# An fp32 attention and two-layer network kernel: first layer in blocks of 416 and 448 tokens, and GpSimd held at every third weight piece

## The chip, the cores and the metric

The kernel runs on one core of a Trainium2 chip. The metric is the device time of one execution in microseconds; lower is better. A core has TensorE (PE, matrix products), VectorE (DVE), ScalarE (ACT), GpSimd (POOL) and SyncE (SP, which here issues the DMAs). They run independently and wait for each other on semaphores.

## What is computed

```python
def reference(q, k, v, moe_w_gate, moe_w_val, moe_w_out, moe2_w_in, moe2_w_out, moe2_alpha):
    x = attention(q, k, v)                      # 4 x 8 heads, 576 positions, 64 wide
    x = x.transpose(0, 2, 1, 3).reshape(2304, 512)
    g = x @ moe_w_gate                          # 512 x 1536
    x = (g / (1 + exp(-g)) * (x @ moe_w_val)) @ moe_w_out
    h = x @ moe2_w_in                           # 512 x 2048
    return (max(h, 0) + moe2_alpha * min(h, 0)) @ moe2_w_out
```

The attention is the sum of two parts: one over keys and queries averaged in fours, and a local one over the neighbours less than 4 positions away. All of it is float32.

## The kernel before

**Precision.** Each factor of the large products is split into a high part in TensorE's reduced float32 form and a low part that holds the rest. A product takes three matmuls: high by high, high by low, low by high (PARTS and products(), L1092; outputs(), L1120; outputs2(), L1137). In all of them 128 x 128 of one operand are loaded first and the other streams past, as many columns as its width.

**Layer one** takes the 2,304 tokens in six blocks with widths SPANS (L70) and first tokens STARTS. A block has 12 steps, one for each 128 hidden units, and a step has three places: the gate product (12 matmuls), the value product (12 matmuls) and the output product of the step before (12 matmuls, accumulated in four banks of PSUM over the block). Between them the other engines work: ScalarE takes the tanh of the gate (L702), VectorE forms gated (L924) and hidden (L929), ScalarE copies hidden to h_hi (high_part, L674) and VectorE subtracts for h_lo (low_part, L914). The output product waits for h_lo_ready. The three weight pieces of step c are 3c (gate), 3c+1 (value) and 3c+2 (output), 36 in all, each 128 x 512.

**Weights.** SyncE loads a piece; for pieces 2 and up ScalarE copies its high part (first_weights_hi, L625), and GpSimd subtracts for the low part w_lo (low_part and split_rest, L520), in the order of the pieces. TensorE waits on w_ready, which counts them. GpSimd also normalises the attention weights of each unit (normalise, L536 and L539); how many pieces come ahead of each unit is set by `ready` in the loop over WORK.

**Attention** for 288 tokens (TB, half a sequence) and two heads is one unit. Four units make a half of x, rows k = 0 to 3 of the tiles x_hi and x_lo. The first half's units run at the start; those of the other seven are woven between the places of blocks 0 to 4, at the places of SCORED_IN, and that order is the same on every engine.

**The ring.** x_hi and x_lo hold, for each k, RING = 1,008 columns. Half a of x is written at the column that x_at() gives, block j reads from HOMES[j]. A block of 432 columns spans one and a half halves. Half 3 is the one of which block 2 reads the first 144 columns and block 3 the rest, and the two blocks lie in different parts of the ring: so it is written in two parts of 144 columns, 288 columns apart (x_at with a == 3).

**Layer two** reads x again from DRAM in six blocks of 384 tokens, in turns from the x2 tiles "even" and "odd". The odd pair shares its memory with x_hi and x_lo, the even pair with the attention's tiles behind y_sb. A block has 16 steps of 12 product matmuls of 384 columns and 9 output matmuls of 512 columns (L1137, where the weights stream and h is loaded).

The order is written by hand in each engine's block:

```python
SPANS = (288, 288, 432, 432, 432, 432)
HOMES = (432, 720, 0, 576, 0, 432)
...
            def split_rest(j):
                low_part(j, w_hi_copied, j - POOL_PIECES + 1)
...
                ready = min(max(EARLY_PIECES + unit.scored + 3, done), P1)
                for j in range(done, ready):
                    split_rest(j)
                done = ready
                normalise(unit.q, unit.q % PAIRS, 1)
```

Of the kernel before, what the change touches and what calls it, by code (L numbers as in the profile page):

```python
# [5 lines left out]
ALU = mybir.AluOpType  # L6
ACT = mybir.ActivationFunctionType
AX_X = mybir.AxisListType.X
F32 = mybir.dt.float32
# [12 lines left out]
TB = SEQ // 2  # L22
# [41 lines left out]

POOL_PIECES = 2
EARLY_PIECES = 6
EARLY_HI = 12
POOL_AVERAGES = 2
BANK = 512
SPANS = (288, 288, 432, 432, 432, 432)  # L70
STARTS = (0, 288, 576, 1008, 1440, 1872)
HOMES = (432, 720, 0, 576, 0, 432)
RING, WIDEST = 1008, max(SPANS)
NL1 = len(SPANS)
STEPS1 = NL1 * C1
TB2 = 384
# [9 lines left out]
class Unit:  # L86

    def __init__(self, q, block, place, following):
        narrow = SPANS[block] == TB
        self.q, self.scored = q, PLACES * block + place  # L90
# [28 lines left out]
def halves_for(j):  # L119

    return -(-(STARTS[j] + SPANS[j]) // TB)


def build(nc, qk, vwin, vsrc, w1, w2, alpha, out, y_t):
    with ExitStack() as ctx:
        def sem(name):
            return ctx.enter_context(nc.semaphore(name))

        def sb(name, shape, dt=F32, where=ctx):
            return where.enter_context(nc.sbuf_tensor(name, shape, dt))  # L130
# [4 lines left out]
        def bank(n):  # L135
            return ps[:, n * BANK:(n + 1) * BANK]

        y_ps = [[bank(m)[:, 0:span] for m in range(KC)] for span in SPANS]
        gate_ps, val_ps = [bank(4)[:, 0:span] for span in SPANS], [bank(5)[:, 0:span] for span in SPANS]

# [36 lines left out]
        with ExitStack() as early:  # L177
            sb("first_pieces", [128, EARLY_HI, PIECE], where=early)
            qk_early = [sb(f"qk_early{k}", [128, QK_W], where=early) for k in range(2, PAIRS)]
# [20 lines left out]
        with ExitStack() as first_x:  # L200
            x_hi = sb("x_hi", [128, KC, RING], F32R, where=first_x)
            x_lo = sb("x_lo", [128, KC, RING], F32R, where=first_x)
        with ExitStack() as second_x:
            x2_hi_odd = sb("x2_hi_odd", [128, KC, TB2], F32R, where=second_x)
            x2_lo_odd = sb("x2_lo_odd", [128, KC, TB2], F32R, where=second_x)
        sb("x_space", [128, 2 * KC * RING])
# [47 lines left out]
        x_f32 = ([x_f32_one] + x_f32_early, [x_f32_one] * PAIRS)  # L254
# [62 lines left out]
        x_hi_ready = sem("x_hi_ready")  # L317
        x_lo_ready = sem("x_lo_ready")
# [7 lines left out]
        h_lo_ready = sem("h_lo_ready")  # L326
# [12 lines left out]

        def x_at(ring, k, a):  # L340

            if a == 3:
                return ring[:, k, TB:3 * TB].rearrange("p (n s) -> p n s", n=2)[:, :, 0:TB // 2]
            first = (432, 720, 0, None, 720, 0, 288, 576)[a]
            return ring[:, k, first:first + TB]

        def x_from(tile, a):

            return tile[:, :].rearrange("p (n s) -> p n s", n=2) if a == 3 else tile[:, :]

        def second_layer(token_block):
            for j in range(NB2):
# [7 lines left out]
        def _(sp):  # L360
# [3 lines left out]
            def load_vwin(q, r):  # L364
                sp.dma_start(vwin_sb[0][r][:, :, :], vwin[bass.ds(q, 1), :, :, :].rearrange("a p t d -> (a p) t d")).then_inc(vwin_in[r], 16)
# [44 lines left out]
            def store_y(j):  # L410
                sp.wait_ge(y02_copied, 2 * j + 6)
                sp.wait_ge(y13_copied, 2 * j + 6)
                sp.dma_start(y_t[:, :, STARTS[j]:STARTS[j] + SPANS[j]].rearrange("k p s -> p k s"), y1_sb[j]).then_inc(y_stored, 16)

# [15 lines left out]
            for k in range(PAIRS):  # L430
# [3 lines left out]
                load_vwin(k, k)  # L434
            load_pieces(FIRST_LOADS, EARLY_PIECES)
            sp.dma_start(alpha_sb[:, :], alpha[:, :]).then_inc(alpha_in, 16)
# [3 lines left out]
            refill_vwin(0)  # L440
            load_pieces(EARLY_PIECES, EARLY_PIECES + 3)
            refill_vwin(1)
            load_pieces(EARLY_PIECES + 3, EARLY_LOADS)

# [37 lines left out]
        def _(pool):  # L482
# [34 lines left out]
            def low_part(at, hi_done, n):  # L517

                pool.wait_ge(hi_done, n)
                nc.gpsimd.tensor_tensor(w_lo[:, at, :], w_raw(at), w_hi[:, at, :].bitcast(F32), ALU.subtract).then_inc(w_ready, 1)  # L520

            def split_rest(j):
                low_part(j, w_hi_copied, j - POOL_PIECES + 1)

            def split_piece(j):
# [36 lines left out]
            for k in range(PAIRS - 1):  # L562
                split_x_lo(k)
            for j in range(POOL_PIECES, EARLY_PIECES):
                split_rest(j)
            done = EARLY_PIECES
            for unit in WORK:
                ready = min(max(EARLY_PIECES + unit.scored + 3, done), P1)
                for j in range(done, ready):
# [9 lines left out]
        def _(act):  # L579
# [35 lines left out]

            def split_x_hi(a, k, mode):
                act.wait_ge(x_added, PAIRS * a + k + 1)
                nc.scalar.copy(x_at(x_hi, k, a), x_from(x_f32[mode][k], a)).then_inc(x_hi_ready, 1)

# [119 lines left out]
        def _(dve):  # L741
# [91 lines left out]

            def split_x_lo(a, k, mode):
                dve.wait_ge(x_hi_ready, PAIRS * a + k + 1)
                nc.vector.tensor_tensor(x_at(x_lo, k, a), x_from(x_f32[mode][k], a), x_at(x_hi, k, a).bitcast(F32), ALU.subtract).then_inc(x_lo_ready, 1)

            def copy_out(j, steps):

# [126 lines left out]
        def _(pe):  # L966
# [176 lines left out]
            def first_block(j):  # L1143
                x_here = [ring[:, :, HOMES[j]:HOMES[j] + SPANS[j]] for ring in (x_hi, x_lo)]
                for p in range(PLACES):
# [82 lines left out]
```

## Time and profile before

| What | Before |
|---|---|
| median of 3 runs | 958.58 us (957.58 to 960.65) |
| the profiled execution's own time | 959.2 us |
| its span, from the first to the last instruction | 957.4 us |
| TensorE busy | 937.7 us, 98% of the span |
| VectorE / ScalarE / GpSimd busy | 504.4 / 279.6 / 140.9 us |
| mean granted clock of TensorE | 0.989 of full speed |

The profile is one execution, taken by the hardware. A row of a timeline says when an instruction (or several like it, x2) started, how long it took, and in brackets how long its engine had stood idle and what ended that. A matmul's recorded duration reaches into the next one's, so the spacing of their starts says what one costs. The chain of waits follows the work that ended last back to the start. L520 is line 520 of the kernel before.

### The profile page before, as it was taken

To read this page: it belongs to the slowest core of one execution; us is meant where nothing else is said; L and a number is where in the kernel's file an instruction comes from. 1 tells how busy PE (TensorE), PEld (TensorE's weight loads), DVE (VectorE), ACT (ScalarE), POOL (GpSimd) and SP (SyncE) were. 2 spreads that over 40 slices of the span, in tenths; PEclk is the share of its full clock that TensorE was granted. 3 is DMA by queue.
4 is the path that set the end of the run, shared out by engine and by line. 5 is a ranking of instruction groups with operands and counts; after the bars stand their busy time and mean duration, and the time that the engine had idled before them with its cause. 6 is when DMAs were issued, how large, how long until landed. Compare 5 with 4: busy or idle time off the path is not lost.

```text
span 957.4 us, 19243 instructions
## 1 busy us (share of the span) xinstructions
PE 937.7 (98%) x7944; PEld 861.9 (90%) x7944; DVE 504.4 (53%) x996; ACT 279.6 (29%) x707; POOL 140.9 (15%) x167
## 2 busy tenths in 40 slices
PE   4899999999999999999999999999999999999998
PEld 3899999999999999999999999998999998999897
DVE  8899777545466765444324245444444444444443
ACT  4566444322233433332134321111111111111111
POOL 7876010000011000000036430000000000000000
PEclk7899999999999999999999999999999999999999
DMA  9763323211122213110232320010100100100000
GB/s 270 240 199 105 104 81 108 78 48 41 41 70 84 90 66 92 54 34 2 75 128 100 120 72 1 12 55 1 66 0 1 66 2 0 66 1 1 34 1 34
DMA packets 31077, 63.24 MB, mean 66 GB/s; under 512 B 3344, under 2 KB 13584, under 8 KB 30992
## 3 DMA queue, kind: packets, MB, share of 16 engines
q1 hardware_dynamic: 30992, 62.02, 20.2%
q8 instruction: 64, 1.05, 0.4%
q14 instruction: 21, 0.17, 0.1%
HBM read 52.57 MB, written 9.44 MB: 65 GB/s over the span
## 4 chain that ended last, share of the span: by engine, by line
PE 95%; DVE 1%; DMA 1%; ACT 1%; SPq 1%; issue 0%; POOL 0%; DVEq 0%; ACTq 0%
PE ps L1092 53%; PE ps L1137 21%; PE ps L1120 16%; PE ps L1040 2%; PE ps L976 1%; DMA vsrc_early<-vsrc 1%; PE ps L986 1%; PE ps L1053 1%; PE ps L1024 1%; DVE h_lo L914 1%; SPq L369 0%; PE ps L1101 0%; ACT turned_early L604 0%; SPq L362 0%; ACT turned_one L604 0%
## 5 line engine op out<-in xcount | busy, mean ns | idle before, releaser
L674 ACT CAST h_hi<-hidden 128x384 fp32r<-128x384 f32 (+2 forms) x168 | 86.2, 513 | 426.0 <-DVE hidden L947 335.7
L1092 PE MATMUL ps<-x_hi,w_hi 128*128 128x432 f32 (+1 forms) x573 | 199.0, 347 | 0.0
L1092 PE MATMUL ps<-x_hi,w_lo 128*128 128x432 f32 (+1 forms) x573 | 193.2, 337 | 0.0
L1092 PE MATMUL ps<-x_lo,w_hi 128*128 128x432 f32 (+1 forms) x573 | 193.0, 337 | 0.0
L914 DVE TENSOR_TENSOR h_lo<-hidden,h_hi 128x384 fp32r<-128x384 f32 (+2 forms) x168 | 108.7, 647 | 72.3 <-ACT h_hi L674 72.3
L945 DVE TENSOR_SCALAR gated<-ps,alpha_sb 128x384 f32<-128x384 f32 x96 | 59.3, 618 | 165.3 <-PE ps L1092 165.3
L1137 PE MATMUL ps<-w_hi,h_hi 128*128 128x512 f32 x288 | 113.8, 395 | 0.4 <-DVE h_lo L914 0.4
L1137 PE MATMUL ps<-w_lo,h_hi 128*128 128x512 f32 x288 | 113.7, 395 | 0.0
L1137 PE MATMUL ps<-w_hi,h_lo 128*128 128x512 f32 x288 | 113.5, 394 | 0.0
L1092 PEld LDWEIGHTS ps<-x_hi,w_hi 128*128 128x128 f32 x573 | 107.9, 188 | 5.2 <-issue 0.2
L1092 PEld LDWEIGHTS ps<-x_lo,w_hi 128*128 128x128 f32 x573 | 107.9, 188 | 2.9
L1092 PEld LDWEIGHTS ps<-x_hi,w_lo 128*128 128x128 f32 x573 | 107.7, 188 | 3.0
L924 DVE SCALAR_TENSOR_TENSOR gated<-gated,ps 128x432 f32<-128x432 f32 (+1 forms) x72 | 39.5, 548 | 129.2 <-ACT gated L702 129.2
L520 POOL TENSOR_TENSOR w_lo<-w_home,w_hi 128x512 fp32r<-128x512 f32 x68 | 89.5, 1335 | 98.1 <-ACT w_hi L669 86.3
L1120 PE MATMUL ps<-h_hi,w_hi 128*128 128x432 f32 (+1 forms) x288 | 99.6, 346 | 2.6 <-DVE h_lo L914 2.5
L1120 PE MATMUL ps<-h_lo,w_hi 128*128 128x432 f32 (+1 forms) x288 | 97.4, 338 | 0.0
L1120 PE MATMUL ps<-h_hi,w_lo 128*128 128x432 f32 (+1 forms) x288 | 97.2, 338 | 0.0
L702 ACT ACTIVATE gated<-ps 128x432 f32<-128x432 f32 (+1 forms) x72 | 35.4, 491 | 145.8 <-PE ps L1092 145.8
L1137 PEld LDWEIGHTS ps<-w_lo,h_hi 128*128 128x128 f32 x288 | 54.1, 188 | 13.0
L929 DVE SCALAR_TENSOR_TENSOR hidden<-gated,ps 128x432 f32<-128x432 f32 (+1 forms) x72 | 39.8, 553 | 48.5 <-PE ps L1092 47.9
L1092 PE MATMUL ps<-x_lo_even,w_hi 128*128 128x384 f32 x192 | 64.9, 338 | 0.0
L1092 PE MATMUL ps<-x_hi_even,w_lo 128*128 128x384 f32 x192 | 64.8, 338 | 0.0
(140 smaller groups left out, 1431.8 us busy)
## 6 DMA issues: line engine op xcount, KB each, us to landing
w_home<-w SPq DMA_DIRECT2D x68, 256.0 KB, 3.8
qk<-qk SPq DMA_DIRECT2D x30, 436.0 KB, 3.7
vsrc_one<-vsrc SPq DMA_DIRECT2D x58, 144.0 KB
vwin<-vwin SPq DMA_DIRECT2D x30, 192.0 KB, 2.4
x_raw<-y_t SPq DMA_DIRECT2D x6, 768.0 KB, 5.5
out<-y_sb SPq DMA_DIRECT2D x5, 768.0 KB, 4.0
y_t<-y_sb SPq DMA_DIRECT2D x4, 864.0 KB, 4.6
y_t<-y_sb SPq DMA_DIRECT2D x2, 576.0 KB, 4.0
```

What stands on the lines that cost most here:

```text
L520: nc.gpsimd.tensor_tensor(w_lo[:, at, :], w_raw(at), w_hi[:, at, :].bitcast(F32), ALU.subtract).then_inc(w_ready, 1)
L674: nc.scalar.copy(h_hi[r][:, 0:width], hidden[r][:, 0:width]).then_inc(h_hi_ready, 1)
L702: nc.scalar.activation(gated[:, 0:span], gate_ps[j], ACT.Tanh, scale=0.5).then_inc(tanh_ready, 1)
L914: nc.vector.tensor_tensor(h_lo[r][:, 0:width], hidden[r][:, 0:width], h_hi[r][:, 0:width].bitcast(F32), ALU.subtract).then_inc(h_lo_ready, 1)
L924: nc.vector.scalar_tensor_tensor(out=gated[:, 0:span], in0=gated[:, 0:span], scalar=1.0, in1=gate_ps[j], op0=ALU.add, op1=ALU.mult).then_i ...
L929: nc.vector.scalar_tensor_tensor(out=hidden[r][:, 0:span], in0=gated[:, 0:span], scalar=0.5, in1=val_ps[j], op0=ALU.mult, op1=ALU.mult).th ...
L945: nc.vector.tensor_scalar(gated[:, 0:TB2], pre_ps[r], 0.0, alpha_sb[:, c:c + 1], ALU.min, ALU.mult).then_inc(gated_ready, 1)
L976: last = nc.tensor.matmul(local_ps(mode, k, e)[GK * i:GK * i + SCORED, t * GK:(t + 1) * GK], qk_sb[mode][k][rows, first:first + SCORED], q ...
L1040: nc.tensor.matmul(att_ps(mode, k, r)[rows, t * ROW_Q:(t + 1) * ROW_Q].rearrange("p (i q) -> p i q", q=GQ), vwin_sb[mode][k][keys, t, rows ...
L1092: mm = nc.tensor.matmul(out_ps, w[:, piece, 128 * k:128 * k + 128], x_parts[low][:, k, :], start=(k == 0 and n == 0), stop=(k == KC - 1 an ...
L1120: mm = nc.tensor.matmul(y_ps[j][m], w[:, piece, 128 * m:128 * m + 128], (h_lo if low else h_hi)[c % 2][:, 0:SPANS[j]], start=(c == 0 and n ...
L1137: mm = nc.tensor.matmul(banks[m], (h_lo if low else h_hi)[c % 2][:, 128 * m:128 * m + 128], w[:, piece, :], start=(c == 0 and n == 0), sto ...
```

## The change

Blocks 2 to 5 of layer one have 416, 448, 448 and 416 tokens. The ring has 1,024 columns, the homes move, and half 3 now lies in one piece: block 2 reads columns 160 to 576, the first 288 of them half 2 and the last 128 the head of half 3, and block 3 goes on at 576. A spacer of 16 numbers (64 bytes) moves the odd x2 tiles. The buffers that have the width of the widest block (h_hi, h_lo, gated, hidden, y_sb) become 448 wide, and with them the tiles behind move. On GpSimd, each piece from 9 on whose number is divisible by 3 also waits for h_lo of step (piece - 9) / 3.

```diff
+PACED = 9
-SPANS = (288, 288, 432, 432, 432, 432)
-STARTS = (0, 288, 576, 1008, 1440, 1872)
-HOMES = (432, 720, 0, 576, 0, 432)
-RING, WIDEST = 1008, max(SPANS)
+SPANS = (288, 288, 416, 448, 448, 416)
+STARTS = (0, 288, 576, 992, 1440, 1888)
+HOMES = (448, 736, 160, 576, 0, 448)
+HALVES_AT = (448, 736, 160, 448, 736, 0, 288, 576)
+RING, WIDEST = 1024, max(SPANS)
...
         with ExitStack() as second_x:
+            sb("odd_start", [128, 16], where=second_x)
             x2_hi_odd = sb("x2_hi_odd", [128, KC, TB2], F32R, where=second_x)
...
         def x_at(ring, k, a):
 
-            if a == 3:
-                return ring[:, k, TB:3 * TB].rearrange("p (n s) -> p n s", n=2)[:, :, 0:TB // 2]
-            first = (432, 720, 0, None, 720, 0, 288, 576)[a]
-            return ring[:, k, first:first + TB]
-
-        def x_from(tile, a):
-
-            return tile[:, :].rearrange("p (n s) -> p n s", n=2) if a == 3 else tile[:, :]
+            return ring[:, k, HALVES_AT[a]:HALVES_AT[a] + TB]
...
             def split_rest(j):
+                if j >= PACED and j % 3 == 0:
+                    pool.wait_ge(h_lo_ready, (j - PACED) // 3 + 1)
                 low_part(j, w_hi_copied, j - POOL_PIECES + 1)
...
-                nc.scalar.copy(x_at(x_hi, k, a), x_from(x_f32[mode][k], a)).then_inc(x_hi_ready, 1)
+                nc.scalar.copy(x_at(x_hi, k, a), x_f32[mode][k][:, :]).then_inc(x_hi_ready, 1)
```

GpSimd's order from piece 2 on, in block 0 of layer one, before (w_lo is the low part of one piece; local_one and down belong to the normalising of a unit):

```order
L520 TENSOR_TENSOR w_lo<-w_home,w_hi 128x512 [waits w_hi_copied] x8
L536 TENSOR_TENSOR local_one<-local_one,row_inv 128x192 [waits inv_ready]
L539 TENSOR_TENSOR down<-down,row_inv 72x8x36
L520 TENSOR_TENSOR w_lo<-w_home,w_hi 128x512 [waits w_hi_copied] x6
L536 TENSOR_TENSOR local_one<-local_one,row_inv 128x192 [waits inv_ready]
L539 TENSOR_TENSOR down<-down,row_inv 72x8x36
L520 TENSOR_TENSOR w_lo<-w_home,w_hi 128x512 [waits w_hi_copied] x6
```

And with the change:

```order
L516 TENSOR_TENSOR w_lo<-w_home,w_hi 128x512 [waits w_hi_copied] x7
L516 TENSOR_TENSOR w_lo<-w_home,w_hi 128x512 [waits w_hi_copied,h_lo_ready]
L534 TENSOR_TENSOR local_one<-local_one,row_inv 128x192 [waits inv_ready]
L537 TENSOR_TENSOR down<-down,row_inv 72x8x36
L516 TENSOR_TENSOR w_lo<-w_home,w_hi 128x512 [waits w_hi_copied] x2
L516 TENSOR_TENSOR w_lo<-w_home,w_hi 128x512 [waits w_hi_copied,h_lo_ready]
L516 TENSOR_TENSOR w_lo<-w_home,w_hi 128x512 [waits w_hi_copied] x2
L516 TENSOR_TENSOR w_lo<-w_home,w_hi 128x512 [waits w_hi_copied,h_lo_ready]
L534 TENSOR_TENSOR local_one<-local_one,row_inv 128x192 [waits inv_ready]
L537 TENSOR_TENSOR down<-down,row_inv 72x8x36
L516 TENSOR_TENSOR w_lo<-w_home,w_hi 128x512 [waits w_hi_copied] x2
L516 TENSOR_TENSOR w_lo<-w_home,w_hi 128x512 [waits w_hi_copied,h_lo_ready]
L516 TENSOR_TENSOR w_lo<-w_home,w_hi 128x512 [waits w_hi_copied] x2
```

The order of the work is the same; the eighth piece of the first run (piece 9), the third and the sixth of the second (pieces 12 and 15) and so on now wait for h_lo_ready too.

TensorE's order where block 1's last outputs end and block 2's first gate product begins, before:

```order
L1120 MATMUL ps<-h_hi,w_hi 128x288
L1120 MATMUL ps<-h_lo,w_hi 128x288
L1120 MATMUL ps<-h_hi,w_lo 128x288
L1092 MATMUL ps<-x_hi,w_hi 128x432 [waits gated_ready,w_ready,x_lo_ready,x_hi_ready]
L1092 MATMUL ps<-x_lo,w_hi 128x432
```

And with the change:

```order
L1118 MATMUL ps<-h_hi,w_hi 128x288
L1118 MATMUL ps<-h_lo,w_hi 128x288
L1118 MATMUL ps<-h_hi,w_lo 128x288
L1090 MATMUL ps<-x_hi,w_hi 128x416 [waits gated_ready,w_ready,x_lo_ready,x_hi_ready]
L1090 MATMUL ps<-x_lo,w_hi 128x416
```

Nothing moved there; the matmuls of block 2 have 416 columns, not 432, and wait for the same semaphores. The line numbers are those of the changed kernel.

## Rows read from the trace of the kernel before

**Rows 1.** The page: the span, and each engine's busy time.

```profile
span 957.4 us, 19243 instructions
...
PE 937.7 (98%) x7944; PEld 861.9 (90%) x7944; DVE 504.4 (53%) x996; ACT 279.6 (29%) x707; POOL 140.9 (15%) x167
```

**Rows 2.** Waits of TensorE, 20 to 958 us: total, times, longest us.

```profile
PE ps L1120 <- DVE h_lo L914: 2.5, 2, 1.8
```

**Rows 3.** Timeline of TensorE, 26 to 58 us: start, duration, [idle before <- releaser].

```profile
37.74 0.37 PE L1120 MATMUL ps<-h_hi,w_hi 128*128 128x288 f32 x1 [0.75 <-DVE h_lo L914]
...
43.54 0.30 PE L1092 MATMUL ps<-x_hi,w_lo 128*128 128x288 f32 x1
45.63 0.37 PE L1120 MATMUL ps<-h_hi,w_hi 128*128 128x288 f32 x1 [1.80 <-DVE h_lo L914]
45.84 0.29 PE L1120 MATMUL ps<-h_lo,w_hi 128*128 128x288 f32 x1
```

**Rows 4.** Timeline of VectorE, 24 to 62 us: h_lo of steps 0 to 3.

```profile
36.28 1.31 DVE L914 TENSOR_TENSOR h_lo<-hidden,h_hi 128x288 fp32r<-128x288 f32 x1 [0.41 <-ACT h_hi L674]
...
41.19 4.30 DVE L914 TENSOR_TENSOR h_lo<-hidden,h_hi 128x288 fp32r<-128x288 f32 x1
...
49.21 1.31 DVE L914 TENSOR_TENSOR h_lo<-hidden,h_hi 128x288 fp32r<-128x288 f32 x1 [0.41 <-ACT h_hi L674]
...
53.73 2.22 DVE L914 TENSOR_TENSOR h_lo<-hidden,h_hi 128x288 fp32r<-128x288 f32 x1
```

**Rows 5.** Timeline of GpSimd, 0 to 110 us.

```profile
36.00 2.74 POOL L520 TENSOR_TENSOR w_lo<-w_home,w_hi 128x512 fp32r<-128x512 f32 x2 [0.22 <-ACT w_hi L625]
39.08 0.51 POOL L536 TENSOR_TENSOR local_one<-local_one,row_inv 128x192 f32<-128x192 f32 x1 [0.35 <-DVE row_inv L811]
...
40.17 5.00 POOL L520 TENSOR_TENSOR w_lo<-w_home,w_hi 128x512 fp32r<-128x512 f32 x4
48.92 2.74 POOL L520 TENSOR_TENSOR w_lo<-w_home,w_hi 128x512 fp32r<-128x512 f32 x2 [3.75 <-ACT w_hi L625]
52.01 0.51 POOL L536 TENSOR_TENSOR local_one<-local_one,row_inv 128x192 f32<-128x192 f32 x1 [0.34 <-DVE row_inv L811]
...
56.04 2.68 POOL L520 TENSOR_TENSOR w_lo<-w_home,w_hi 128x512 fp32r<-128x512 f32 x2 [0.41 <-ACT w_hi L625]
```

**Rows 6.** Timeline of GpSimd, 41.5 to 43.9 us: pieces 11 and 12.

```profile
41.42 2.53 POOL L520 TENSOR_TENSOR w_lo<-w_home,w_hi 128x512 fp32r<-128x512 f32 x2
```

**Rows 7.** Timeline of ScalarE, 25 to 60 us: the high part of piece 12.

```profile
41.70 0.62 ACT L625 CAST w_hi<-w_home 128x512 fp32r<-128x512 f32 x1
```

**Rows 8.** Chain of waits, 0 to 115 us: start, us, what, matmuls.

```profile
47.46 1.59 PE ps L1092 x12
...
51.69 1.82 PE ps L1120 x12
```

**Rows 9.** Chain of waits, 470 to 500 us, block 5 of layer one.

```profile
470.16 4.69 PE ps L1092 x24
...
498.38 1.76 PE ps L1092 x9
```

**Rows 10.** Chain of waits, 565 to 690 us, layer two.

```profile
568.99 2.12 PE ps L1092 x12
571.11 2.08 PE ps L1137 x9
...
610.99 2.12 PE ps L1092 x12
...
619.38 2.11 PE ps L1092 x12
...
678.27 2.11 PE ps L1092 x12
```

**Rows 11.** Groups of instructions by form: count | busy us, mean ns | idle.

```profile
L1092 PE MATMUL ps<-x_hi,w_hi 128*128 128x432 f32 x384 | 140.4, 366 | 0.0
...
L1120 PE MATMUL ps<-h_hi,w_hi 128*128 128x432 f32 x192 | 69.8, 364 | 0.0
```

More of the change, by code:

```diff
@@ L835, in split_x_lo @@
                 dve.wait_ge(x_hi_ready, PAIRS * a + k + 1)
-                nc.vector.tensor_tensor(x_at(x_lo, k, a), x_from(x_f32[mode][k], a), x_at(x_hi, k, a).bitcast(F32), ALU.subtract).then_inc(x_lo_ready, 1)
+                nc.vector.tensor_tensor(x_at(x_lo, k, a), x_f32[mode][k][:, :], x_at(x_hi, k, a).bitcast(F32), ALU.subtract).then_inc(x_lo_ready, 1)
             def copy_out(j, steps):
```

## The prediction

> **What bounds the kernel now.** I read the page first. TensorE is busy for 937.7 of 957.4 us [rows 1], and its multiplications make up nearly the whole chain of waits. So a change pays in one of two ways only: TensorE stops waiting somewhere, or a matmul follows the one before it sooner. I then read what TensorE waits for after the first 20 us. Of the waits that the change touches only one is large: before its output matmuls it waits for the low part of the hidden activation (h_lo), 2.5 us in two waits of which the longest is 1.8 [rows 2]. TensorE's own timeline gives the place: a product matmul starts at 43.54, the next one, an output matmul of step 1, at 45.63; the smaller wait of 0.75 us ends at 37.74, in step 0 [rows 3]. VectorE's timeline shows why: h_lo of step 1 starts at 41.19 and takes 4.30 us, where those of steps 0, 2 and 3 take 1.31, 1.31 and 2.22 [rows 4]. GpSimd's timeline fits to the hundredth: it forms the low parts of four weight pieces back to back from 40.17 to 45.17, and h_lo ends 0.31 us later, at 45.49. Around the shorter ones it runs only pairs of pieces, from 36.00 and from 48.92 [rows 5]. Both engines subtract two tiles that lie in SBUF.
>
> The Trainium skill describes this: in "SBUF — State Buffer", section "Who interferes with whom", a VectorE instruction with two SBUF inputs and a GpSimd instruction that reads SBUF exclude each other, and whoever issues first holds the shared ports for its whole instruction. The trace agrees that one waits, but not on how long: by that rule h_lo would wait for the piece in progress only.
>
> **The hold on GpSimd.** Pieces 9, 12, 15 and so on wait for h_lo of steps 0, 1, 2. The changed order shows the first burst cut into seven pieces and a held one, the second into two, a held one, two, a held one.
>
> *Piece 12, step 1.* Pieces 10 and 11 run as before; piece 12 is the third of the four. Piece 11 starts at 41.42 and two pieces from there take 2.53 us [rows 6], so it ends at about 41.42 + 1.27 = 42.69. There GpSimd now stands still, h_lo needs its 0.31 us, and is ready at about 43.0 in place of 45.49. TensorE could start its output matmul one spacing of 0.13 us after 43.54, at 43.67: h_lo is then ready 0.6 us early and the wait is gone. The gain is 45.63 - 43.67 = 1.96 us, and the first matmul after the wait is followed after 0.21 us, not 0.13, which gives 0.08 more [rows 3]: **2.0 us**. It isn't given back in the next step: VectorE gains 2.5 us there, more than TensorE's 2.0, so its lead grows.
>
> *What stands behind the waiting piece.* Piece 12 itself was waiting for ScalarE's high part until 41.70 + 0.62 = 42.32 [rows 7]; held, it runs from about 43.1 to 44.4, piece 13 to 45.7. Piece 12 is a gate weight of step 4, and TensorE starts that step's gate only behind the outputs that it begins at 51.69 [rows 8], 49.7 after the gain: over 5 us are left. Behind piece 13 come piece 14, which waited for ScalarE until 48.92 anyway [rows 5], and the normalising of the next attention unit.
>
> *The other holds.* Piece 9 is held until h_lo of step 0 ends at 37.59 instead of starting near 37.2: either way it ends before the normalising at 39.08 [rows 5]; cost 0, gain 0. The 0.75 us of step 0 stays, because pieces 6 to 8 aren't held and h_lo waits for piece 8. Piece 15 is the second of the pair at 48.92, held until 50.52 [rows 4, 5]; it then ends near 51.9, and GpSimd's next work starts at 52.01 [rows 5]. Piece 18 started at 56.04, after h_lo of step 3 had ended at 55.95: already late enough, and pieces 16 and 17 hold that h_lo up as before. This pair of steps repeats to piece 35, so the later holds change nothing. If TensorE's slack there were gone, each h_lo of 2.22 us would cost up to 1.8 us; in the trace TensorE doesn't wait for one.
>
> **Widths 416 and 448.** The instruction counts stay; 4 x (288 + 144) = 1,728 matmuls of 432 columns, three times 384 and three times 192 [rows 11], become 864 of 416 and 864 of 448, with the same sum of columns. What I need is the spacing of two new widths, and no row has it. The rows give for 432 columns four steps of 36 matmuls in 498.38 - 470.16 = 28.22 us, 196.0 ns each, 0.454 ns a column [rows 9]; for 384 columns 2.12 / 12 = 176 ns, 0.459 a column, for 512 columns 2.08 / 9 = 231 ns, 0.451 [rows 10]; for 288 columns 1.59 / 12 = 132.5 ns, 0.460 [rows 8]. A pair now takes 392.0 ns. At the cheapest rate it would take 864 x 0.4514 = 390.0 (864 x -2.0 ns = -1.7 us), at the dearest 864 x 0.460 = 397.4 (+4.7 us). I take 0: both new widths lie 16 columns from 432, the nearest row, and a slope cancels in the pair. Block by block it doesn't cancel: block 2 gets shorter by 432 x 7 ns = 3 us and block 3 longer by as much, with attention units of unchanged size in both. VectorE and ScalarE are 16 columns shorter or longer with it, which their idle time hides.
>
> **New places.** Adding up the tiles, x_hi began at a multiple of 128 bytes; its rows for the four k were 4,032 bytes apart, so every second one started on an odd multiple of 64 bytes, and with the homes 432 and 720 the other ones. Now rows are 4,096 apart and all homes are multiples of 128 bytes. In layer two the x2 tiles, both at even multiples of 64 before, now both start on odd ones; the spacer of 16 numbers does that for the odd tile and costs no time. The nearest rows are the two x2 tiles of before, whose starts differ by 128 bytes modulo 256: even block, ten steps in 610.99 - 568.99 = 42.00 us, 4.200 each; odd block, fourteen in 678.27 - 619.38 = 58.89, 4.206 each [rows 10]. A place moves the time by a thousandth, either way: I take 0. The lower bound is that the narrow matmuls come down to the rate of the cheapest row: 1,152 of 384 columns by 176 - 173.3 = 2.7 ns (3.1 us) and 864 of 288 columns by 2.5 ns (2.2 us); the upper bound stands under the rivals.
>
> The copies of half 3 of x lose their split form and keep 288 columns; DMAs stay in number and order. All of that costs 0, hidden by idle time of VectorE and ScalarE.
>
> **Sum.** 959.2 us (the profiled execution) - 2.0 + 0 + 0 = 957.2. The median of the runs, 958.58, is 0.6 lower than that execution, so I predict **956.6**. A measurement of this kernel tells about 0.3%, 2.9 us, from no change; this forecast is below that.
>
> **The rivals.**
> *Matmuls follow each other sooner as well.* With even places every matmul of layer one and the narrow ones of layer two could approach the cheapest rate: at most 1.7 + 3.1 + 2.2 = 7.0 us, with the hold 9.0, 949.6; at half of it 953.1. For it: 0.459 against 0.451 a column is no law of width alone. Against it: the two x2 places differ by 0.006 us a step. Chance 0.35, for 950 to 955.5.
> *The hold frees nothing.* If h_lo waits for one instruction only, its 4.30 us has another cause and piece 12's hold gains 0: 958.6. This is the skill's lock taken at its word. The end 0.31 us behind a burst of four speaks against it; chance 0.07.
> *Slower: a product pays for its odd start.* If each matmul that reads x2 from an odd multiple of 64 bytes took up 64 bytes more, 16 columns at 0.459, that is 7.3 ns x 1,152 = 8.5 us: 956.6 + 8.5 = 965.1. It decides once the 96 steps of layer two grow by over 2.0 / 96 = 0.02 us each. Against it: block 5 read odd and even rows by turns, at 0.454 a column. The same skill page, under "Specifications (TRN2)", names lines of 16 bytes, by which no place here would matter; no run here shows it. Chance 0.07.
> *Slightly dearer widths*, up to +2.9 us: 957.5 to 959.5, chance 0.08.
>
> **How the numbers follow.** The forecast, 955.5 to 957.5, has 0.43. The range of 8 in 10 goes from 952.0 to 959.5: it leaves out the slower rival and the far end of the faster one. Faster by over 0.3% means under 955.7: 0.35 and a little of the forecast, 0.38. Slower: 0.07. Same: 0.55.
>
> **What would show it.** Right: h_lo of step 1 takes about 1.8 us and TensorE no longer waits before the outputs of step 1; a wait of about 0.75 remains in step 0; 12 outputs of 416 columns take about 2.27 us and of 448 about 2.44; steps of layer two stay at 4.20. Wrong: h_lo of step 1 still takes 4 us; TensorE waits for a low part of a weight; or the steps of layer two move by 0.02 us or more, which makes the places, not the hold, the larger part.

## The result, and the profile after

| What | Before | After |
|---|---|---|
| median | 958.64 us (957.58 to 960.65, 4 runs) | 951.05 us (950.30 to 951.81, 4 runs) |
| the profiled execution's own time | 959.2 us | 951.09 us |
| its span | 957.4 us | 949.0 us |
| TensorE busy | 937.7 us | 931.3 us |

The ratio is 0.9918, with an interval of 0.9900 to 0.9936: 7.6 us faster, where 2.0 were forecast. The page of the changed kernel, its span and the busy times, beside [rows 1]:

```profile
span 949.0 us, 19252 instructions
...
PE 931.3 (98%) x7944; PEld 857.6 (90%) x7944; DVE 504.5 (53%) x996; ACT 279.3 (29%) x707; POOL 140.2 (15%) x167
```

TensorE issues the same 7,944 matmuls and is busy for 6.4 us less. Waits that go away don't change busy time much; matmuls that follow each other sooner do.

First the place that the forecast was about. TensorE's waits for h_lo after 20 us, in all, times, longest (us), beside [rows 2] (L1118 and L1135 are outputs() and outputs2() now):

```profile
PE ps L1118 <- DVE h_lo L912: 0.9, 1, 0.9
...
PE ps L1135 <- DVE h_lo L912: 0.5, 1, 0.5
```

VectorE's timeline, steps 0 to 3 and the first instruction of the next attention units, beside [rows 4]:

```profile
35.69 1.31 DVE L912 TENSOR_TENSOR h_lo<-hidden,h_hi 128x288 fp32r<-128x288 f32 x1 [0.42 <-ACT h_hi L672]
...
40.81 1.82 DVE L912 TENSOR_TENSOR h_lo<-hidden,h_hi 128x288 fp32r<-128x288 f32 x1
...
47.01 1.33 DVE L912 TENSOR_TENSOR h_lo<-hidden,h_hi 128x288 fp32r<-128x288 f32 x1 [0.41 <-ACT h_hi L672]
48.63 1.09 DVE L805 TENSOR_SCALAR row_padded<-row_sum 128x8 f32<-128x8 f32 x1
...
51.76 2.22 DVE L912 TENSOR_TENSOR h_lo<-hidden,h_hi 128x288 fp32r<-128x288 f32 x1
...
60.81 1.09 DVE L805 TENSOR_SCALAR row_padded<-row_sum 128x8 f32<-128x8 f32 x1
```

The hold did what was said: h_lo of step 1 takes 1.82 us instead of 4.30, and the wait of 1.80 us [rows 3] is gone. Only the one of step 0 is left, 0.94 us.

Then layer two. The chain of waits of the changed kernel there (start, us, what; L1090 is products(), L1135 outputs2()), beside [rows 10]:

```profile
566.86 2.08 PE ps L1090 x12
568.94 2.05 PE ps L1135 x9
...
624.73 2.08 PE ps L1090 x12
626.81 2.05 PE ps L1135 x9
```

The first pair lies in an even block, the second in an odd one, and they are alike. From 566.86 to 624.73 there are 14 steps, 57.87 us, 4.134 each, where before they took 4.200 and 4.206. Over 96 steps this is about 96 x 0.07 = 6.7 us.

I took the start of every block from TensorE's matmuls in both traces, and the differences of these starts add up to the whole:

| Stretch | Before | After | Difference |
|---|---|---|---|
| up to the first full product of block 0 | 31.90 | 31.02 | -0.9 |
| block 0 (steps 0 to 11) | 68.86 | 68.41 | -0.45 |
| block 1 | 72.58 | 72.59 | 0 |
| blocks 2 to 5, together | 374.23 | 373.81 | -0.4 |
| layer two, from its first matmul to the end of the kernel | 409.85 | 403.21 | -6.6 |

Together they are -8.4 us, the difference of the two spans, 957.4 and 949.0. In layer two the first five blocks, 67.2 to 67.5 us each before and 66.1 to 66.3 after, and the last one with its tail get shorter by 1.06 to 1.15 each.

The first full product also starts 0.6 to 0.9 us sooner or later between executions of kernels that are the same up to there; I claim nothing of that row. Block 0 repeats better when it is counted from the first matmul of products() in it, the last quarter of its first gate product (29.74 and 29.15 us). It then takes 71.01 us before and 70.28 with the change, 0.7 less. In the five kernels of this document that have no hold it takes 70.98 to 71.04, in the six with the hold on every third piece 70.23 to 70.36.

TensorE's granted clock was lower at the start of the profiled execution before (0.74 in its first 24 us, 0.83 in the next 24, against 1.0 with the change). It has no part in the rows below the first: the kernel with the hold alone, next section, was granted 1.0 throughout, and a block of its layer two takes 67.21 to 67.46 us, as before.

So two questions stood: what in layer two got cheaper, though nothing in it was changed but addresses; and why block 0, which lost a wait of 1.8 us, is only 0.5 to 0.7 shorter.

### The profile page after: what moved, and what is told of

The parts are those of the page before. It is cut to its first block, busy times and chain, and to the rows that moved or that the text cites. A ratio compares the mean times of both kernels' runs of the same rounds, so it can differ in the third digit from the quotient of the medians.

```text
span 949.0 us, 19252 instructions
## 1 busy us (share of the span) xinstructions
PE 931.3 (98%) x7944; PEld 857.6 (90%) x7944; DVE 504.5 (53%) x996; ACT 279.3 (29%) x707; POOL 140.2 (15%) x167
## 4 chain that ended last, share of the span: by engine, by line
PE 90%; DVE 4%; issue 2%; ACT 1%; DMA 1%; SPq 1%; POOL 0%; DVEq 0%; ACTq 0%
PE ps L1090 50%; PE ps L1135 21%; PE ps L1118 14%; PE ps L1038 1%; PE ps L974 1%; DMA vsrc_early<-vsrc 1%; PE ps L984 1%; PE ps L1051 1%; PE ps L1022 1%; DVE v_d_one L768 1%; DVE row_padded L805 1%; DVE gated L922 0%; DVE h_lo L912 0%; DVE neg_max L796 0%; SPq L365 0%
## 5 line engine op out<-in xcount | busy, mean ns | idle before, releaser
L672 ACT CAST h_hi<-hidden 128x384 fp32r<-128x384 f32 (+3 forms) x168 | 86.3, 513 | 419.6 <-DVE hidden L945 329.4
L1090 PE MATMUL ps<-x_hi,w_hi 128*128 128x416 f32 (+2 forms) x573 | 199.1, 347 | 0.0
L1090 PE MATMUL ps<-x_lo,w_hi 128*128 128x416 f32 (+2 forms) x573 | 193.1, 337 | 0.0
L1090 PE MATMUL ps<-x_hi,w_lo 128*128 128x416 f32 (+2 forms) x573 | 193.1, 337 | 0.0
L912 DVE TENSOR_TENSOR h_lo<-hidden,h_hi 128x384 fp32r<-128x384 f32 (+3 forms) x168 | 106.4, 633 | 72.2 <-ACT h_hi L672 72.2
L1135 PE MATMUL ps<-w_hi,h_hi 128*128 128x512 f32 x288 | 112.3, 390 | 0.5 <-DVE h_lo L912 0.5
L1135 PE MATMUL ps<-w_hi,h_lo 128*128 128x512 f32 x288 | 112.6, 391 | 0.0
L1090 PEld LDWEIGHTS ps<-x_hi,w_hi 128*128 128x128 f32 x573 | 107.6, 188 | 5.5 <-DVE gated L922 0.3
L1135 PE MATMUL ps<-w_lo,h_hi 128*128 128x512 f32 x288 | 112.4, 390 | 0.0
L1090 PEld LDWEIGHTS ps<-x_hi,w_lo 128*128 128x128 f32 x573 | 107.7, 188 | 3.3
L1090 PEld LDWEIGHTS ps<-x_lo,w_hi 128*128 128x128 f32 x573 | 107.8, 188 | 2.8
L1118 PE MATMUL ps<-h_hi,w_hi 128*128 128x288 f32 (+2 forms) x288 | 99.7, 346 | 0.9 <-DVE h_lo L912 0.9
L1118 PE MATMUL ps<-h_lo,w_hi 128*128 128x288 f32 (+2 forms) x288 | 96.9, 336 | 0.0
L1118 PE MATMUL ps<-h_hi,w_lo 128*128 128x288 f32 (+2 forms) x288 | 96.9, 336 | 0.0
L927 DVE SCALAR_TENSOR_TENSOR hidden<-gated,ps 128x288 f32<-128x288 f32 (+2 forms) x72 | 39.8, 552 | 48.3 <-PE ps L1090 47.6
L1090 PE MATMUL ps<-x_hi_odd,w_lo 128*128 128x384 f32 x192 | 64.5, 336 | 0.0
L1090 PE MATMUL ps<-x_hi_even,w_lo 128*128 128x384 f32 x192 | 64.5, 336 | 0.0
```

Of the source, the lines that this page charges most:

```text
L672: nc.scalar.copy(h_hi[r][:, 0:width], hidden[r][:, 0:width]).then_inc(h_hi_ready, 1)
L912: nc.vector.tensor_tensor(h_lo[r][:, 0:width], hidden[r][:, 0:width], h_hi[r][:, 0:width].bitcast(F32), ALU.subtract).then_inc(h_lo_ready, 1)
L927: nc.vector.scalar_tensor_tensor(out=hidden[r][:, 0:span], in0=gated[:, 0:span], scalar=0.5, in1=val_ps[j], op0=ALU.mult, op1=ALU.mult).th ...
L1090: mm = nc.tensor.matmul(out_ps, w[:, piece, 128 * k:128 * k + 128], x_parts[low][:, k, :], start=(k == 0 and n == 0), stop=(k == KC - 1 an ...
L1118: mm = nc.tensor.matmul(y_ps[j][m], w[:, piece, 128 * m:128 * m + 128], (h_lo if low else h_hi)[c % 2][:, 0:SPANS[j]], start=(c == 0 and n ...
L1135: mm = nc.tensor.matmul(banks[m], (h_lo if low else h_hi)[c % 2][:, 128 * m:128 * m + 128], w[:, piece, :], start=(c == 0 and n == 0), sto ...
```

## The experiments

**What lies where.** The places below are the starts of tiles in bytes modulo 256, from adding up the tiles in the order of their allocation. They count the first tile, the weights' high part, as 128, which no trace shows; the distances between tiles don't depend on it. Before: h_hi of the two buffers at 128 and 64, h_lo at 0 and 192 (each is 1,728 bytes long, 64 short of a multiple of 256); x2 of even blocks at 0, of odd blocks at 128. After: all four h tiles at 128 (1,792 bytes each, a multiple of 256), x2 of both at 192. The split weights are at 128 in both. The change thus moved two things in layer two, the streamed x2 and the loaded h.

**The hold alone.** The kernel before with the hold added.

```diff
             def split_rest(j):
+                if j >= 9 and j % 3 == 0:
+                    pool.wait_ge(h_lo_ready, (j - 9) // 3 + 1)
```

> The kernel before with the hold on GpSimd alone; widths, ring and tiles as before. Theory 'VectorE takes over': in the changed kernel the steps of block 0 behind the freed wait grew from about 5.8 to 6.4 us every second step, and the chain there runs on VectorE. So the hold gives 2.0 us in step 2 and loses most of it again by the end of block 0: 0.3 to 0.9 us faster in all, about 958.0, block 0 about 0.5 us shorter. Rival 'the full wait': nothing is given back, 2.0 us faster, 956.6, the steps behind it keep their 5.8 to 6.0 us.

Measured: 958.58 us (957.59 to 959.70, 11 runs) against 959.91 for before (20 runs), ratio 0.9986, interval 0.9977 to 0.9996: 1.3 us, a little more than was expected. TensorE's wait goes, as in the changed kernel. Of it block 0 keeps 0.6 (68.27 us), as expected; in block 1 one step takes 0.6 more than before, and VectorE waits 2.2 us for a transfer of queries and keys there (1.7 before). The hold is not where the 7.6 us come from.

**The change without the hold.** The changed kernel, and only the wait on GpSimd taken out.

```diff
             def split_rest(j):
-                if j >= PACED and j % 3 == 0:
-                    pool.wait_ge(h_lo_ready, (j - PACED) // 3 + 1)
```

> The changed kernel without the hold; widths and places of the change stay. Theory 'places carry it': layer two keeps its steps of 4.13 us, and only the hold's net part is lost: 951.4 to 952.0, and step 1's h_lo takes about 4.3 us again. Rival 'the hold matters more': 953 or more.

Measured: 952.36 us (5 runs) against 959.91, ratio 0.9928 (0.9914 to 0.9942), -7.55 us. Steps of layer two are 4.13 us, block 0 is 69.16. Nearly the whole gain is there without the hold. The ratio, 0.9928 beside 0.9918 for the change, leaves about 1 us for it, within the noise of both; block 0, 0.75 longer than in the changed kernel, says the same more surely.

**Only x2 moved.** The kernel before, its widths and ring unchanged, with spacers so that both x2 pairs start at 192.

```diff
         with ExitStack() as second_x:
+            sb("odd_start", [128, 16], where=second_x)
...
+        sb("even_start", [128, 48])
         x2_hi = [sb("x2_hi_even", [128, KC, TB2], F32R), x2_hi_odd]
```

> The kernel before with the two x2 tiles of layer two moved, by spacers of 64 and 192 bytes, to the places modulo 256 bytes that they have in the changed kernel; nothing else moves. Theory 'the streaming operand's place': the 12 product matmuls fall from 2.11 to about 2.08 us, the 9 output matmuls, which stream weights that have not moved, stay at 2.08 to 2.10; steps near 4.17, 3 us faster. Rival 'the loaded operand's place' (h): no change, 4.20. Rival 'the pace of one group carries on into the next': both groups fall, steps 4.13, 6.7 us faster.

Measured: 956.53 us (9 runs) against 959.91, ratio 0.9967 (0.9956 to 0.9979), -3.4 us. Its chain in layer two:

```profile
600.48 2.10 PE ps L1139 x9
602.58 2.08 PE ps L1094 x12
604.66 2.08 PE ps L1139 x9
```

The 12 products are down from 2.11 to 2.08 us; the 9 outputs still take 2.10 and 2.08 by turns, as the h buffers take turns. A step is 4.17.

**Only h moved.** The kernel before, with each h tile 16 numbers longer, so that all four start at 128; x2 stays at 0 and 128.

```diff
-        h_hi = [sb(f"h_hi{r}", [128, WIDEST], F32R) for r in range(2)]
-        h_lo = [sb(f"h_lo{r}", [128, WIDEST], F32R) for r in range(2)]
+        h_hi = [sb(f"h_hi{r}", [128, WIDEST + 16], F32R) for r in range(2)]
+        h_lo = [sb(f"h_lo{r}", [128, WIDEST + 16], F32R) for r in range(2)]
...
+        sb("even_start", [128, 64])
         x2_hi = [sb("x2_hi_even", [128, KC, TB2], F32R), x2_hi_odd]
```

> The kernel before with 64 bytes more behind each of the four h tiles, so that all four start at the same place modulo 256 bytes as in the changed kernel; the x2 tiles keep their places modulo 512 bytes. Theory 'streaming operand': layer two's 9 output matmuls, which only load h, stay at 2.08 to 2.10, and the 12 products too; layer one's output matmuls, which stream h, get a little faster, under 1 us in all. Rival 'loaded operand': the 9 outputs fall to 2.05 and the products stay at 2.11: steps 4.16, 3.5 us faster.

Measured: 956.17 us (6 runs) against 959.91, ratio 0.9961 (0.9947 to 0.9975), -3.7 us. Its chain, first in an even block, then in an odd one:

```profile
601.64 2.10 PE ps L1093 x12
603.75 2.06 PE ps L1138 x9
...
618.31 2.10 PE ps L1093 x12
620.41 2.08 PE ps L1138 x9
```

Now the outputs are cheaper, 2.06 and 2.08, and no longer go by turns; the products stay at 2.10. Blocks 2 to 5 of layer one, where h streams, are 373.5 us together, 0.7 less than before. There are two effects, mainly one of x2 on the products and one of h on the outputs. By the traces, layer two is 3.1 us shorter with x2 moved, 2.8 with h moved, and 6.6 with both (the next experiment), 0.7 more than the sum.

**Both moved, nothing else.** The last two edits together: widths 432, ring of 1,008, no hold.

```diff
+            sb("odd_start", [128, 16], where=second_x)
...
+        h_hi = [sb(f"h_hi{r}", [128, WIDEST + 16], F32R) for r in range(2)]
+        h_lo = [sb(f"h_lo{r}", [128, WIDEST + 16], F32R) for r in range(2)]
...
+        sb("even_start", [128, 112])
```

> The kernel before with both moves of the two experiments before: x2 tiles and h tiles at the places modulo 256 bytes of the changed kernel, widths 432, no hold. Theory 'places carry layer two': products 2.08 and outputs 2.05 us, steps 4.13, layer two 6.7 us shorter than before; 953 against 959.9. Rival 'the two moves overlap': steps stay near 4.16, 956.

Measured: 951.94 us (5 runs) against 959.67 for before (9 runs), ratio 0.9924 (0.9911 to 0.9938), -7.7 us. Its chain in layer two is that of the changed kernel, 4.13 a step:

```profile
568.02 2.08 PE ps L1094 x12
570.10 2.05 PE ps L1139 x9
572.15 2.08 PE ps L1094 x12
```

Blocks 2 to 5 take 373.5 us with 432 columns, 373.3 with 416 and 448 and no hold. So the widths, the ring and the homes together bring nothing that can be measured (they were not tried one by one): a few numbers more in the allocation do.

**Other places for x2.** The changed kernel with x2 of even and odd blocks at 0 and 128, and at 64 and 0; h stays at 128. One execution each, read by their traces.

```diff
-            sb("odd_start", [128, 16], where=second_x)
+            sb("odd_start", [128, 32], where=second_x)
...
+        sb("even_start", [128, 32])
```

(the second; the first takes odd_start out and puts an even_start of 16)

> The changed kernel with the even x2 tiles at 0 and the odd ones at 128 bytes modulo 256 (both at 192 in the changed kernel; the weights that are loaded against them lie at 128). h is left where the change has it. Theory 'odd multiples of 64 are the good ones for x2': steps above 4.13 in both kinds of block, products near 2.11. Rival 'any one place for all is good': steps stay at 4.13 in both.

> The changed kernel with the even x2 tiles at 64 and the odd ones at 0 bytes modulo 256. Theory 'odd multiples of 64': even blocks keep products of 2.08 and steps of 4.13, odd blocks have dearer ones, 4.16 or more. Rival 'only 192 is good': both dearer.

Measured: 955.07 and 953.12 us. The chain of the second kernel, first an even block (x2 at 64), then an odd one (at 0):

```profile
608.10 2.12 PE ps L1091 x12
610.22 2.04 PE ps L1136 x9
612.26 2.10 PE ps L1091 x12
614.37 2.06 PE ps L1136 x9
```

A step takes 4.16 us with x2 at 64 or at 0, 4.19 at 128 (the odd blocks of the first, 66.99 / 16), 4.13 at 192. The same place at 0 or at 128 costs the same in either kernel's products, 2.10 to 2.11. Where x2 lies also shifts the outputs behind them by up to 0.04 us, so only the whole step compares. Both expectations had a theory that odd multiples of 64 are the cheap places, and the second experiment refutes it: at 64 a step costs as much as at 0, and of the four places only 192 is cheap.

The first kernel has the same places modulo 256 as the one in which only h moved, but not modulo 512 (counted from the weights, its even x2 tiles start 384 bytes past a multiple of 512, there 128), and widths, ring and hold differ. Its blocks of layer two take 66.99 and 66.56 us by turns, as there. That speaks for the places modulo 256 as the ones to look at.

**Other places for h.** The changed kernel with h at 192 (spacer of 16 numbers) and at 64 (spacer of 48); x2 stays at 192.

```diff
         sb("x_space", [128, 2 * KC * RING])
+        sb("h_start", [128, 16])
         h_hi = [sb(f"h_hi{r}", [128, WIDEST], F32R) for r in range(2)]
...
+        sb("even_start", [128, 112])
```

> The changed kernel with all four h tiles 64 bytes further, at 192 modulo 256; x2 stays at 192. Theory 'one place for all four h tiles is what counts': outputs of layer two stay at 2.05. Rival 'the loaded operand must lie at the same place as the streaming weights, 128': outputs rise to 2.08 or more.

> The changed kernel with the four h tiles at 64 modulo 256 bytes (128 in the change), x2 at 192, the weights at 128. In layer two the products stream x2 from 64 bytes past their loaded operand's place and are cheapest so; the outputs stream the weights. Theory 'streaming 64 bytes past the loaded operand is the cheap place in both': outputs at or below 2.05. Rival 'equal places are the cheap ones for the outputs': outputs 2.08 or more.

Measured: 954.47 us for 192, 957.89 for 64, one execution each. The chain of the one with h at 192:

```profile
584.92 2.10 PE ps L1137 x9
587.02 2.08 PE ps L1092 x12
```

At 192 and at 64 the outputs take 2.10 us, at 128 2.05, with the same products. The theory that what counts is by how much the streamed operand starts past the loaded one falls with these two. What is left for the outputs is that of the three places tried (all four tiles at 0 was not) h is cheapest at the very place of the weights that stream past it, 128. For the products that rule doesn't hold: their weights are loaded from 128 too, x2 is cheapest at 192, and at 128 it is dearest. Of the 6.8 us that the kernel with h at 64 is slower than the changed one, layer two is 3.8 and blocks 2 to 5 are 0.5. The other 2.4 are in its start, where TensorE waits 4.9 us for a normalised tile (2.9 in the changed kernel), and one execution doesn't tell whether a place has a part in that.

**The hold on piece 12 only.** The other question, block 0. In the changed kernel VectorE is slower there than TensorE: row_padded, which it does once for every two steps, is at 48.63 and 60.81, 12.18 apart, and takes 1.09 us, where it took 0.87 before. Its GpSimd timeline shows what is new beside it, beside [rows 5]:

```profile
48.42 1.28 POOL L516 TENSOR_TENSOR w_lo<-w_home,w_hi 128x512 fp32r<-128x512 f32 x1 [0.40 <-DVE h_lo L912]
```

That is piece 15, held until h_lo ends, and started just ahead of row_padded, which then ends 0.02 us after it. The experiment leaves the hold on piece 12 alone.

```diff
             def split_rest(j):
-                if j >= PACED and j % 3 == 0:
-                    pool.wait_ge(h_lo_ready, (j - PACED) // 3 + 1)
+                if j == 12:
+                    pool.wait_ge(h_lo_ready, 2)
```

> The changed kernel with the hold on piece 12 alone; pieces 9, 15, 18, 21 and so on go as soon as their high part is there. Theory 'the held second piece of a pair delays VectorE': in the changed kernel row_padded (two engines, one port) takes 1.10 us in place of 0.87 once per attention unit, because the held piece starts 0.2 us later; without it the period of VectorE's chain in block 0 falls from 12.17 to about 11.96 us, block 0 gets 0.8 us shorter, total 950.2 to 950.6 beside 951.3 for the change. Rival: the 12.17 us have another cause, block 0 stays at 68.4.

Measured: 950.04 us (4 runs) against 958.94 for before (7 runs), ratio 0.9908 (0.9892 to 0.9925). VectorE's timeline:

```profile
48.58 0.87 DVE L805 TENSOR_SCALAR row_padded<-row_sum 128x8 f32<-128x8 f32 x1
...
60.55 0.87 DVE L805 TENSOR_SCALAR row_padded<-row_sum 128x8 f32<-128x8 f32 x1
```

The two steps take VectorE 11.97 us, and block 0 is 67.14 us instead of 68.41, 69.19 instead of 70.28 by the other count. The medians of the two kernels lie within each other's noise; block 0, which repeats within 0.15 us by that count, tells them apart. Of the 1.1 us 0.9 lie in the last four pairs of steps, where the holds on pieces 15, 21 and so on act, and 0.2 in steps 0 and 1, where the one on piece 9 does. Without any hold block 0 takes 70.99. So the hold on piece 12 wins 1.8 us there, and the other holds cost 1.1 of them.

**Holds where VectorE needs them.** If GpSimd's bursts are what makes VectorE slow, holds at better pieces should bring block 0 down to what TensorE needs. Pieces 10, 16, 22 and on wait for the h_lo of the step at hand, pieces 12, 18, 24 and 30 for neg_max of the unit, and one piece less comes ahead of each unit.

```diff
-                if j >= PACED and j % 3 == 0:
-                    pool.wait_ge(h_lo_ready, (j - PACED) // 3 + 1)
+                if j >= 10 and j % 6 == 4:
+                    pool.wait_ge(h_lo_ready, (j - 10) // 3 + 2)
+                if j >= 12 and j % 6 == 0:
+                    pool.wait_ge(neg_max_ready, PAIRS + (j - 12) // 6 + 2)
...
-                ready = min(max(EARLY_PIECES + unit.scored + 3, done), P1)
+                ready = min(max(EARLY_PIECES + unit.scored + 2, done), P1)
```

> The changed kernel with other holds: pieces 10, 16, 22, 28, 34 wait for the h_lo that collides with them (steps 1, 3, 5, 7, 9), pieces 12, 18, 24, 30 for the row maxima of the next attention unit, and one piece more goes behind each normalising (9, 15, 21, ...). Theory 'VectorE's waits for the shared port set block 0': h_lo of the odd steps falls from 2.2 to about 0.5 us, the chain on VectorE gets shorter than TensorE's 11.8 us for two steps, block 0 falls to 66.6 to 67.4 us, total about 950. Rival 'it only moves the waits': other VectorE instructions wait for the pieces instead, block 0 stays at 68.4 or grows.

Measured: 949.15 us (948.50 to 950.49, 4 runs) against 958.94, ratio 0.9900 (0.9884 to 0.9917). VectorE's timeline, h_lo of steps 1 and 3 and the unit's row_padded:

```profile
39.66 0.59 DVE L914 TENSOR_TENSOR h_lo<-hidden,h_hi 128x288 fp32r<-128x288 f32 x1
...
49.80 0.58 DVE L914 TENSOR_TENSOR h_lo<-hidden,h_hi 128x288 fp32r<-128x288 f32 x1
...
57.91 0.88 DVE L807 TENSOR_SCALAR row_padded<-row_sum 128x8 f32<-128x8 f32 x1
...
69.68 0.88 DVE L807 TENSOR_SCALAR row_padded<-row_sum 128x8 f32<-128x8 f32 x1
```

Two steps now take 11.77 us, which is TensorE's own pace (5.77 + 5.99 for the two kinds of step), and block 0 is 66.65 us, 1.8 less than in the changed kernel. One piece also comes behind the normalising that came ahead of it, so this run doesn't tell what the holds bring without that. VectorE's busy time, with the same instructions, falls by 10 us, which are waits for GpSimd inside its own instructions:

```profile
PE 928.6 (98%) x7944; PEld 856.9 (91%) x7944; DVE 494.4 (52%) x996; ACT 280.1 (30%) x707; POOL 141.5 (15%) x167
```

It has the lowest median of all that ran, 9.8 us under before. Its interval overlaps with that of the changed kernel, 0.9900 to 0.9936, which was timed against other runs of before; block 0 tells them apart.

## Why the prediction was wrong, step by step

**What bounds it, and the hold: right in its mechanism, wrong in what it keeps.** The wait of 1.8 us went, by the numbers given: h_lo of step 1 takes 1.82 us, TensorE waits for no low part of a weight, and step 2 takes 5.88 us instead of 7.90, 2.0 less. Block 0 gives back 1.4 us of it (steps 4 to 11 take 48.56 us instead of 47.40, and steps 0 and 1 together 9.85 instead of 9.65). Two steps of the prediction failed there.

The larger one is "*The other holds*", priced at 0. In the kernel with the hold on piece 12 alone steps 4 to 11 take 47.69 us, and steps 0 and 1 9.64: so the other holds cost 0.9 and 0.2. Piece 15 was checked against "GpSimd's next work starts at 52.01". But that work waits for VectorE's row_inv [rows 5], and row_inv for row_padded, which piece 15 holds up: 0.22 us more in every period of VectorE, 12.18 instead of 11.96. The hold on piece 9 does the same to the first row_padded, 1.10 us instead of 0.87.

The smaller one is "It isn't given back in the next step: VectorE gains 2.5 us there, more than TensorE's 2.0, so its lead grows." The lead, from the end of h_lo to the start of its outputs, grew to 0.7 us in step 1, but in step 2 it was 0.85 us where before it was 1.10: neg_max, which met no piece before and took 0.17 us, took 0.82 beside the held piece 12 and piece 13. And row_padded of the kernel before comes every 11.96 us:

```profile
50.82 0.87 DVE L807 TENSOR_SCALAR row_padded<-row_sum 128x8 f32<-128x8 f32 x1
...
62.78 0.87 DVE L807 TENSOR_SCALAR row_padded<-row_sum 128x8 f32<-128x8 f32 x1
```

VectorE needed 11.96 us for two steps where TensorE needs 11.76. Behind its long wait TensorE had VectorE's lead to live on: 1.60, 1.44, 1.30 and 1.20 us in steps 3, 5, 7 and 9 before. With the change it is 1.08 and then 0.92 in each, and the slower engine sets the pace. The last four pairs of steps of block 0 take 11.81, 11.80, 11.85 and 11.94 us before, 12.02, 12.18, 12.17 and 12.19 after, and 11.83 to 11.97 in the kernel with the hold on piece 12 alone. That is 1.2 us given back, of which 0.3 go to this step and 0.9 to the other holds. I had checked each held piece against GpSimd's next work and against TensorE, but not against what VectorE does beside it.

**Widths 416 and 448: right.** 12 outputs of 416 columns take 2.24 us and of 448 2.44, 24 products 4.48 and 4.86, as in these rows of the changed kernel's chain (block 4, then block 5), beside 4.69 for 24 products of 432 [rows 9]:

```profile
441.98 4.86 PE ps L1090 x24
446.84 2.44 PE ps L1118 x12
...
472.07 4.48 PE ps L1090 x24
476.55 2.24 PE ps L1118 x12
```

24 products of either width are 9.34 us together, two times 4.69 is 9.38: 1.7 ns a pair less. Over the four blocks little of that is left: they are 0.4 us shorter in all, and the two kernels without a hold and with h at 128 that differ in the widths, the ring and the homes have 373.5 and 373.3 us there. Zero was the right value.

**New places: the step that made the number wrong.** "A place moves the time by a thousandth, either way: I take 0." It moved a step of layer two by 1.6%, 6.6 us in all against a term of 0. Three things were wrong in it. The two x2 places of before, 0 and 128, were taken as a sample of what places do; at those two the products happen to cost the same (2.105 and 2.106 us in one kernel with h at 128), while 192 gives 2.081 and 64 gives 2.120. Second, only the streamed x2 was costed. That h_hi and h_lo move too stood in the change ("with them the tiles behind move") and has no term in the sum, though they are loaded for 864 matmuls and it is worth 2.8 us alone and 3.5 on top of the move of x2. Third, the lower bound let only narrow matmuls get cheaper and held those of 512 columns for the cheapest row, so that the nearest row was taken for a floor; they fell from 2.08 to 2.10 us for nine down to 2.05, which is 3.8 of the 6.6 us. The products gave the other 2.8.

The rule of the Trainium skill in "SBUF — State Buffer", section "Specifications (TRN2)", that a line has 16 bytes, was cited for the view that no place here would matter. The runs disagree with that reading: every place tried is a multiple of 64 bytes, and a step goes from 4.13 to 4.21 us with it.

**The rivals.** "Matmuls follow each other sooner as well" (0.35) is the one whose range came true, in part by luck. Its reason, "even places", can't be that of layer two, where x2 moved to odd multiples of 64. Of its 3.9 us for layer one (1.7 + 2.2) the traces show 0.4 in blocks 2 to 5 and none in block 1; of its 3.1 for the products of layer two they show 2.8; and the 3.8 of the outputs it left out. As to the slower rival, "Slower: a product pays for its odd start" had the sign turned round, since x2 on an odd multiple of 64 is the cheapest in the one case (192) and no dearer in the other (64). "The hold frees nothing" fell with the run of the hold alone. It was what the Trainium skill says in "SBUF — State Buffer", section "Who interferes with whom", taken at its word: whoever issues first holds the shared ports for its whole instruction. The prediction read that as: and no longer. The measured waits go both ways. In step 1 h_lo waited through four pieces that followed each other without a gap (4.30 us), and with the burst cut after two it took 1.82; in step 3 it waited through both pieces of a pair. But in steps 0 and 2 it waited for one piece only, as the rule has it, though the next one stood ready: in step 2 of the kernel before h_lo ends at 50.52, 0.31 us behind the first piece of its pair (50.21), and the second takes 1.50 us instead of 1.28. The prediction read only the longer waits.

**The signs.** The prediction named the one that came: steps of layer two that move by 0.02 us or more make the places the larger part. They moved by 0.07. Of the right signs, 12 outputs of 416 columns take 2.24 us where 2.27 were said, and the wait in step 0 is 0.94 where 0.75 were said.

**The range.** It ended at 952.0, 0.95 above the result. The faster rival, by its own price, reached to 949.6, and the range cut that end off; after the two terms above that had no row behind them, it should have stayed in.

## What to carry to other kernels

A change of buffer widths moves every tile behind it: list, before predicting, each operand that TensorE loads or streams with its start modulo 256 bytes before and after, and treat an unseen place as unknown, not as the mean of those seen. In a kernel whose TensorE is 98% busy, a spacer of 64 bytes is a cheap experiment that can be worth more than a reordering, as here. And when a wait goes, compare the periods of the engines behind it: the gain lasts only as far as the next slowest engine keeps TensorE's pace.

## What the runs showed of the hardware

- **Places of TensorE's operands in SBUF.** 12 products of 384 columns and 9 outputs of 512 columns take together 4.133 us with x2 at 192 modulo 256 bytes, 4.160 at 0 and 64, 4.187 at 128 (h at 128). With x2 at 192, h at 128 gives 4.133, h at 64 and 192 4.17 to 4.18. Why, no run tells: neither "both operands at one place" nor "the streamed one 64 bytes past the loaded one" fits products and outputs alike.
- **GpSimd beside VectorE.** h_lo, a VectorE instruction with two SBUF inputs (0.41 to 0.45 us alone), took 4.30 us beside four pieces, 2.22 and 1.82 beside fewer, 0.58 beside the end of one. Whether it is let in between two pieces that follow each other at once varies, and regularly. In block 0 of the 13 traces it was let in all 34 times that VectorE had stood idle just before it (0.05 to 0.42 us), and then the next piece took 1.5 us instead of 1.3. It waited for the rest of the burst all 60 times that it came straight behind another VectorE instruction. Why, no run tells.
- **One input of 8 columns waits as well.** row_padded, 128x8 from 128x8, takes 0.17 us with GpSimd idle and 0.87 to 1.10 beside a piece; neg_max, 72x2, 0.17 and 0.8 to 1.3. Unlike h_lo, neg_max was let in between pieces each time: in the trace before it ends at 34.55, 0.02 us behind a piece, and the next piece, which follows at once, runs to 35.77.
